# Fused attention, experts and MLP on one core: the attention's work put in another order on three engines

## The chip, the cores and the metric

One core of one Trainium2 chip runs the whole program. The metric is the device time of one execution in microseconds (us); lower is better. TensorE multiplies and transposes, ScalarE (ACT) and VectorE (DVE) read its results from the eight PSUM banks, GpSimd (POOL) works on SBUF, and SyncE (SP) issues all DMAs. Each engine works through its own list of instructions in the order in which they are written.

## The reference

```
def sm_attn(qq, kk, vv):
    s = scale * np.matmul(qq, kk.transpose(0, 1, 3, 2))
    s = s - np.max(s, axis=-1, keepdims=True)
    a = np.exp(s)
    a = a / (np.sum(a, axis=-1, keepdims=True) + 1e-09)
    return np.matmul(a, vv)
p_packed = sm_attn(p, k, v)              # 32 packed queries per head
out = sm_attn(q, p_packed, p_packed)     # q, k, v: (4, 8, 576, 64)
...
x = out as (2304, 512); logits = x @ w_gate; P = exp(logits), 8 rounds of row and column scaling
out += P[:, e:e+1] * (relu(x @ w1[e]) @ w2[e])    # 8 experts, hidden 1024
h = x @ w_in; r = relu(h); out = (s * r * r + b) @ w_out   # hidden 2048
```

## The kernel before

Attention goes batch by batch, b = 0 to 3, and two batches are in flight at any time. All that TensorE has to turn round (transpose) is cut into *units*, and a unit fills one PSUM bank: `("p", b, 0)` the packed queries; `("k", b, 0..5)` and `("q", b, 0..5)` four heads by one chunk of tokens each (the third chunk is a short tail); `("e", b, 0..2)` the exponentials of the first softmax; `("pp", b, 0)` the packed values; `("a", b, 0..2)` the weights of the second softmax, which are the attention's result for the experts. The list `UNITS` holds their order. Unit n goes to bank `TR[n % 3]`, and TensorE may write it only when unit n-3 has been copied out (`wait_evacuated(pe, [unit - 3])` in `transposes`). So three units are in flight, and one late copy holds up every turn that follows.

Between the turns stand the products of each batch, in this order of need: `scores1(b, Q)` (packed queries by keys, Q = 0, 1); VectorE's `max1`; ScalarE's `exp1`; `turn_e`; `packed(b)` (80 small matmuls, weights by values); VectorE's `inverse1` and `normalise1`; `turn_packed`; ScalarE's `packed_values`; `scores2(b, c)` for three chunks c; VectorE's `off_max2`; ScalarE's `exp2`; VectorE's `inverse2`; GpSimd's `normalise2`; `turn_a(b, c)`; and `a_chunk(b, c)` on ScalarE (high part) and then on VectorE (low part). `packed_gates`, `gates_of_packed`, `lo_of_packed` and `first_products` prepare gate logits and the first expert group. After the attention comes `hidden(0, 0, 0, 0)` and a long part that is the same in both kernels: 32 expert groups and 8 MLP groups.

The order is written out by hand, once for each engine: the calls in the TensorE block, those in the ScalarE block, those in the VectorE block, and `order_of_units()`, with one pattern for b = 1 and 2. `BY_ACT` fixes who copies: ScalarE copies every unit but `("k", b, 3)`. SyncE loads `q[b + 1]`, the packed queries and `k[b + 2]` when the last unit of `q[b]` has been turned, and `v[b + 1]` after `packed(b)`.

Of the kernel before, what the change touches and what calls it, by code (L numbers as in the profile page):

```python
# [12 lines left out]
P = 128  # L13
# [5 lines left out]
def attention_moe_mlp(nc, q, k, v, p, w_gate, w1, w2, w_in, w_out, s_, b_, out):  # L19
    B, H, S, D = q.shape  # L20
    NPACK = p.shape[2]
# [34 lines left out]
    with ExitStack() as ctx:  # L56
# [127 lines left out]
        ppT_ready = sem("ppT_ready")  # L184
# [103 lines left out]
        def order_of_units():  # L288

            def parts(what, b, some):  # L290
                return [(what, b, n) for n in some] if 0 <= b < B else []
            order = parts("k", 0, range(3)) + parts("p", 0, [0]) + parts("k", 0, range(3, 6)) + parts("q", 0, range(6))
            order += parts("e", 0, range(3)) + parts("pp", 0, [0]) + parts("p", 1, [0])
            order += parts("k", 1, range(6)) + parts("q", 1, range(6))
            for b in range(1, B - 1):
                order += parts("e", b, range(3)) + parts("p", b + 1, [0]) + parts("k", b + 1, range(3))
                order += parts("pp", b, [0]) + parts("k", b + 1, range(3, 6)) + parts("a", b - 1, [0])
                order += parts("q", b + 1, range(4)) + parts("a", b - 1, [1])
                order += parts("q", b + 1, [4, 5]) + parts("a", b - 1, [2])
            order += parts("e", B - 1, range(3)) + parts("a", B - 2, [0]) + parts("pp", B - 1, [0])  # L300
            order += parts("a", B - 2, [1, 2])
            order += parts("a", B - 1, range(NC))
            return order

        UNITS = order_of_units()

        BY_ACT = [("p", 0), ("k", 0), ("k", 1), ("k", 2), ("k", 4), ("k", 5), ("q", 0), ("q", 1), ("q", 2), ("q", 3),
                  ("q", 4), ("q", 5), ("e", 0), ("e", 1), ("e", 2), ("pp", 0)]
# [115 lines left out]
        def _(sp):  # L424
# [55 lines left out]

            for b in range(B - 1):
# [141 lines left out]
        def _(act):  # L623
# [24 lines left out]
            def evacuate(what, b, part, dst, view):  # L648
                assert (what, part) in BY_ACT
                unit = UNITS.index((what, b, part))  # L650
                copy(dst, view(full(unit))).then_inc(evacuated(unit), 1)
# [12 lines left out]
            def a_chunk(b, c):  # L664

                if b < 0:
                    return
                copy(out_cols(a_hi, b, c), turned_a(full(UNITS.index(("a", b, c))), c)).then_inc(a_hi_ready, 1)

            def packed_values(b):  # L670

                i, unit = b % 2, UNITS.index(("pp", b, 0))
                src = full(unit)[:, 0:QUADS * P]
                copy(ppT[i][:], src).then_inc(ppT_ready, 1)
                copy(pp_parts[0:HALF, :, b * NPACK:(b + 1) * NPACK],
                     src[0:HALF, :].rearrange("d (h n) -> d h n", n=NPACK)).then_inc(evacuated(unit), 1)

            def p_part(b):
                if b < B:
                    evacuate("p", b, 0, pT[b % 2][:], lambda bank_: bank_[:, 0:QUADS * P])  # L680

            def k_part(b, n):
                if b == B:
                    return
# [8 lines left out]
            def q_part(b, n):  # L693
                if b < B:
                    evacuate("q", b, n, *queries_of(b, n))

            k_part(0, 0)
            k_part(0, 1)  # L700
            k_part(0, 2)
            p_part(0)
            k_part(0, 4)
            exp1(0, 0)
            k_part(0, 5)
            q_part(0, 0)
            exp1(0, 1)
            for n in range(1, UNITS_IN):
                q_part(0, n)
            for n in range(3):  # L710
                evacuate("e", 0, n, *turned_e(0, n))
            packed_values(0)
            p_part(1)
            exp2(0, 0)
            k_part(1, 0)
            k_part(1, 1)
            k_part(1, 2)
            exp2(0, 1)
            exp1(1, 0)
            k_part(1, 4)  # L720
            k_part(1, 5)
            exp2(0, 2)
            q_part(1, 0)
            exp1(1, 1)
            for n in range(1, UNITS_IN):
                q_part(1, n)
            for b in range(1, B):
                for n in range(3):
                    evacuate("e", b, n, *turned_e(b, n))
                if b == B - 1:  # L730
                    a_chunk(b - 1, 0)
                    packed_values(b)
                    a_chunk(b - 1, 1)
                    a_chunk(b - 1, 2)
                    break
                p_part(b + 1)
                for n in range(3):
                    k_part(b + 1, n)
                packed_values(b)
                exp1(b + 1, 0)  # L740
                k_part(b + 1, 4)
                k_part(b + 1, 5)
                a_chunk(b - 1, 0)
                exp2(b, 0)
                q_part(b + 1, 0)
                exp1(b + 1, 1)
                q_part(b + 1, 1)
                q_part(b + 1, 2)
                exp2(b, 1)
                q_part(b + 1, 3)  # L750
                a_chunk(b - 1, 1)
                exp2(b, 2)
                q_part(b + 1, 4)
                q_part(b + 1, 5)
                a_chunk(b - 1, 2)
# [16 lines left out]

            first_hi_part(0, 0)
            exp2(B - 1, 0)
            first_hi_part(1, 0)
            exp2(B - 1, 1)
            relu(0, 0, 0, 0)
            exp2(B - 1, 2)
            relu(0, 0, 0, 1)
            first_hi_part(0, 1)  # L780
            first_hi_part(1, 1)
            relu(0, 0, 1, 0)
# [69 lines left out]
        def _(dve):  # L852
# [14 lines left out]
            def evacuate(what, b, part, dst, view):  # L867
                assert (what, part) not in BY_ACT
# [31 lines left out]
            def inverse2(b, c):  # L900
                if b < 0:
                    return
# [6 lines left out]
            def a_chunk(b, c):  # L909

                if b < 0:
                    return
# [6 lines left out]
            def k_part(b, n):  # L919
                if b < B:  # L920
                    evacuate("k", b, n, *keys_of(b, n))

            def lo_of_packed(b):
                unit = UNITS.index(("pp", b, 0))
                wait_evacuated(dve, [unit])
# [12 lines left out]

            max1(0, 0)
            k_part(0, 3)  # L940
            max1(0, 1)
            inverse1(0)
            normalise1(0)
            off_max2(0, 0)
            inverse2(0, 0)
            off_max2(0, 1)
            max1(1, 0)
            k_part(1, 3)
            lo_of_packed(0)
            inverse2(0, 1)  # L950
            off_max2(0, 2)
            dve.wait_ge(wg_ready, 2)
            gates_of_packed(0)
            max1(1, 1)
            inverse2(0, 2)
            inverse1(1)
            for b in range(1, B):
                normalise1(b)
                if b == B - 1:
                    for c in range(NC):  # L960
                        a_chunk(b - 1, c)
                    break
                max1(b + 1, 0)
                k_part(b + 1, 3)
                off_max2(b, 0)
                a_chunk(b - 1, 0)
                max1(b + 1, 1)
                inverse2(b, 0)
                off_max2(b, 1)
                gates_of_packed(b)  # L970
                a_chunk(b - 1, 1)
                off_max2(b, 2)
                inverse2(b, 1)
                inverse2(b, 2)
                a_chunk(b - 1, 2)
                inverse1(b + 1)
                lo_of_packed(b)
# [99 lines left out]

            last = B - 1
            off_max2(last, 0)
            first_lo_part(0, 0)  # L1080
            off_max2(last, 1)
            first_lo_part(1, 0)
            off_max2(last, 2)
            inverse2(last, 0)
            lo_of_packed(last)
            gates_of_packed(last)
            inverse2(last, 1)
            lo_of_hidden(0, 0, 0, 0)
            inverse2(last, 2)
            lo_of_hidden(0, 0, 0, 1)  # L1090
            first_lo_part(0, 1)
            first_lo_part(1, 1)
            lo_of_hidden(0, 0, 1, 0)
            lo_of_hidden(0, 0, 1, 1)
# [81 lines left out]
        def _(pe):  # L1176
# [24 lines left out]
            def turn_p(b):  # L1201
                if b < B:
                    pe.wait_ge(p_in[b % 2], (b // 2 + 1) * 32)
# [24 lines left out]
            def scores1(b, Q):  # L1228
                if b == B:
                    return  # L1230
# [77 lines left out]
            def turn_a(b, c):  # L1308
                if b < 0:
                    return  # L1310
# [327 lines left out]
```

## Time and profile before

| | |
|---|---|
| Time, median of 3 (lowest to highest) | 1775.69 us (1770.3 to 1777.31) |
| The profiled execution: its time, its span | 1775.83 us, 1774.0 us |
| TensorE busy (matmul), share of the span | 1752.3 us, 99% |
| VectorE, ScalarE, GpSimd busy | 913.3, 713.2, 609.4 us |
| Granted TensorE clock, mean | 0.991 |

The time is the span plus 1.8 us around it. Busy time of an engine is the time in which the profile has an instruction on it. For TensorE the ends are modelled, so a stretch that is full of matmuls need not run at its peak, but a gap is a gap. The granted clock is 1.00 at 2.4 GHz and 0.50 at 1.2 GHz. The attention takes the first 100 us of the span.

### The profile page before, as it was taken

The numbers are of one execution on the slowest core, as the hardware profiler recorded it, in microseconds if no ns is written. First come the engines' busy times: TensorE is split into PE (matmuls) and PEld (weight loads), VectorE is DVE, ScalarE is ACT, GpSimd is POOL, SyncE is SP. The second block draws the span as 40 slices with busy tenths as digits, with TensorE's granted clock in tenths as the row PEclk, the third lists the DMA queues.
The fourth block names the chain that finished last, engine by engine and source line by source line (L and its number), as shares of the span: only waits on it lengthen the run. The fifth ranks groups of instructions, "written<-read, shape, count | busy, mean of one in ns | idle before, by whom it ended". The sixth has DMA issues, their size and how long they took to land.

```text
span 1774.0 us, 27319 instructions
## 1 busy us (share of the span) xinstructions
PE 1752.3 (99%) x10257; PEld 1525.5 (86%) x10257; DVE 913.3 (51%) x1361; ACT 713.2 (40%) x1574; POOL 609.4 (34%) x380
## 2 busy tenths in 40 slices
PE   8899999999999999999999999999999999999999
PEld 6688888898889888888988898889888888888887
DVE  3555654544544554455445544544556555555555
ACT  4543446345444434443454345444432322222222
POOL 1153444443444444345344443444431011111100
PEclk8899999999999999999999999999999999999999
DMA  7531112111111121111112111111100000000002
GB/s 218 152 72 37 36 36 59 37 47 37 35 36 35 46 48 35 47 35 35 35 35 59 36 45 37 35 35 36 47 24 24 13 24 25 25 24 24 0 0 106
DMA packets 71776, 78.81 MB, mean 44 GB/s; under 512 B 7984, under 2 KB 59184, under 8 KB 71728
## 3 DMA queue, kind: packets, MB, share of 16 engines
q1 hardware_dynamic: 71728, 78.15, 16.6%
q8 instruction: 33, 0.54, 0.1%
q14 instruction: 15, 0.12, 0.0%
HBM read 73.42 MB, written 4.72 MB: 44 GB/s over the span
## 4 chain that ended last, share of the span: by engine, by line
PE 96%; DVE 2%; ACT 1%; issue 0%; DVEq 0%
PE PS L1178 94%; PE PS L1198 1%; DVE acc L1035 1%; PE PS L1473 0%; DVE gate L1012 0%; ACT acc L625 0%; ACT g_raw L625 0%; DVE stat L896 0%; DVE gate L998 0%; DVE stat L905 0%; DVE a_parts L915 0%; DVE stat L906 0%; DVE stat L875 0%; ACT a_parts L625 0%; DVE acc L897 0%
## 5 line engine op out<-in xcount | busy, mean ns | idle before, releaser
L1178 PE MATMUL PS<-w_hi,h_hi 128*128 128x512 f32 x1440 | 563.5, 391 | 1.3 <-DVE acc L1035 1.3
L1178 PE MATMUL PS<-w_hi,h_lo 128*128 128x512 f32 x1440 | 561.0, 390 | 0.0
L1178 PE MATMUL PS<-w_lo,h_hi 128*128 128x512 f32 x1440 | 560.7, 389 | 0.0
L1040 DVE SCALAR_TENSOR_TENSOR acc<-PS,gate,acc 128x512 f32<-128x512 f32 x504 | 378.0, 750 | 266.9 <-PE PS L1178 266.9
L764 ACT ACTIVATE h_hi<-PS 128x576 fp32r<-128x576 f32 x256 | 167.1, 653 | 676.6 <-PE PS L1178 675.9
L1178 PE MATMUL PS<-a_parts,g_parts 128*128 128x288 f32 x3072 | 438.0, 295 | 0.6 <-DVE g_parts L983 0.6
L1178 PEld LDWEIGHTS PS<-a_parts,g_parts 128*128 128x128 f32 x3072 | 419.4, 188 | 6.0 <-DVE g_parts L983 0.7
L625 ACT ACTIVATE g_raw<-PS 32x256 f32<-32x256 f32 x992 | 373.3, 376 | 14.3 <-PE PS L1178 0.4
L1021 DVE SCALAR_TENSOR_TENSOR h_lo<-PS,h_hi 128x576 fp32r<-128x576 f32 x256 | 193.9, 757 | 324.9 <-ACT h_hi L764 324.9
L1178 PEld LDWEIGHTS PS<-w_hi,h_hi 128*128 128x128 f32 x1440 | 270.3, 188 | 57.5 <-DVE acc L1035 3.9
L1178 PEld LDWEIGHTS PS<-w_hi,h_lo 128*128 128x128 f32 x1440 | 270.3, 188 | 57.5
L1178 PEld LDWEIGHTS PS<-w_lo,h_hi 128*128 128x128 f32 x1440 | 270.4, 188 | 52.8
L542 POOL CAST w_hi<-stage 128x1024 fp32r<-128x1024 f32 (+1 forms) x78 | 77.0, 987 | 381.5 <-PE PS L1178 374.8
L565 POOL CAST g_parts<-g_raw 128x1024 fp32r<-128x1024 f32 x62 | 64.6, 1042 | 390.1 <-ACT g_raw L625 390.1
L544 POOL TENSOR_TENSOR w_lo<-stage,w_hi 128x1024 fp32r<-128x1024 f32 (+1 forms) x78 | 169.9, 2179 | 6.2
L1035 DVE TENSOR_TENSOR acc<-PS,acc 128x512 f32<-128x512 f32 x180 | 124.2, 690 | 54.0 <-PE PS L1178 53.2
L567 POOL TENSOR_TENSOR g_parts<-g_raw,g_parts 128x1024 fp32r<-128x1024 f32 x62 | 148.8, 2400 | 5.0
L836 ACT ACTIVATE mlp_f<-PS 128x512 f32<-128x512 f32 (+1 forms) x80 | 44.5, 556 | 219.9 <-PE PS L1178 219.9
L1178 PE MATMUL PS<-a_parts,w_hi 128*128 128x512 f32 (+1 forms) x320 | 117.9, 368 | 0.0
L1178 PE MATMUL PS<-a_parts,w_lo 128*128 128x512 f32 (+1 forms) x320 | 117.7, 368 | 0.0
L1178 PE MATMUL PS<-g_parts,w_hi 128*128 128x512 f32 (+1 forms) x320 | 117.7, 368 | 0.0
L557 POOL CAST w_hi<-stage 128x1024 fp32r<-128x1024 f32 x40 | 41.7, 1042 | 201.5 <-PE PS L1178 197.1
(127 smaller groups left out, 1086.3 us busy)
## 6 DMA issues: line engine op xcount, KB each, us to landing
stage<-moe_w_dram SPq DMA_DIRECT2D x96, 512.0 KB, 5.0
k_raw<-k_dram SPq DMA_DIRECT2D x8, 512.0 KB, 6.1
q_raw<-q_dram SPq DMA_DIRECT2D x8, 512.0 KB, 5.7
v_raw<-v_dram SPq DMA_DIRECT2D x8, 512.0 KB, 6.1
stage<-moe_w_in_dram SPq DMA_DIRECT2D x16, 256.0 KB, 2.9
stage<-moe_w_out_dram SPq DMA_DIRECT2D x8, 512.0 KB, 3.4
out_dram<-acc SPq DMA_DIRECT2D x16, 256.0 KB, 2.2
p_twice<-p_dram SPq DMA_DIRECT2D x8, 64.0 KB, 4.8
```

Source lines behind the costliest of these rows:

```text
L542: nc.gpsimd.tensor_copy(hi, src).then_inc(w1_ready, 1)
L544: nc.gpsimd.tensor_tensor(lo, src, hi.bitcast(F32), ALU.subtract).then_inc(w1_ready, 1)
L557: nc.gpsimd.tensor_copy(w2_hi[par][:], stage2[:]).then_inc(w2_ready, 1)
L565: nc.gpsimd.tensor_copy(g_hi[par][:, Q], g_raw[Q][:]).then_inc(g_hi_ready, 1)
L567: nc.gpsimd.tensor_tensor(g_lo[par][:, Q], g_raw[Q][:], g_hi[par][:, Q].bitcast(F32), ALU.subtract).then_inc(g_lo_ready, 1)
L625: return nc.scalar.activation(dst, src, ACT.Copy)
L764: nc.scalar.activation(dst.rearrange("p (i n) -> p i n", i=2), src, ACT.Relu).then_inc(h_hi_ready, 1)
L836: nc.scalar.activation(mlp_f[:, slot, f, 0:n], bank(HB + 2 * slot + f, n), ACT.Relu).then_inc(relu_ready, 1)
L1021: nc.vector.scalar_tensor_tensor(out=h_lo[:, f, cols].rearrange("p (i n) -> p i n", i=2), in0=bank(HB + 2 * f, 2 * BANK).rearrange("p (i n ...
L1035: return nc.vector.tensor_tensor(dst, y, dst, ALU.add)
L1040: return nc.vector.scalar_tensor_tensor(out=dst, in0=y, scalar=share, in1=dst, op0=ALU.mult, op1=ALU.add)
L1178: return nc.tensor.matmul(dst, lhsT, rhs, start=start, stop=stop)
```

## The change

Nothing that is computed changes, nor how often. The hand-made patterns go. In their place stand four lists, each for all four batches: `TURNED_UNITS` (the order in which banks are filled), the calls of TensorE, those of ScalarE and those of VectorE. Copies are shared out anew: VectorE keeps units k13, k23 and k33 and also copies k00, k04, q02, q00, e01, q05, k15, e11 and k22 (letter, batch, part); ScalarE takes k03. The high part of the packed values is copied from SBUF in a call of its own, `hi_of_packed`, later in ScalarE's list. Waits are finer: `scores1(b, Q)` waits for its own three key units, `scores2(b, c)` for the packed values and for the two query units of its chunk. SyncE waits apart for the turned packed queries and keys. `first_products(0, 0)` and `(1, 0)` move ahead of the last batch's `scores2`, `packed_gates(3)` behind the first `hidden`.

```diff
+        TURNED_UNITS = """
+            p00 k00 k02 k01 k05 k03 k04 q02 q03 e00 q00 e01 e02 q01 q04 q05 p10 k12 k11 pp00 k10 k13
+            k14 k15 q15 q12 q13 q10 k20 q14 k25 e10 q11 e11 e12 k23 k21 p20 k22 k24 q25 pp10 a00 q23
+            q24 q22 a01 q21 e20 e21 e22 q20 p30 a02 k32 k31 k30 k34 pp20 k33 a10 k35 q35 q30 a11 q31
+            e30 e31 q32 e32 q33 q34 a12 a20 pp30 a21 a22 a30 a31 a32
+        """.split()
+        UNITS = [(name[:-2], int(name[-2]), int(name[-1])) for name in TURNED_UNITS]
...
             for b in range(B - 1):
-                sp.wait_ge(tr_full, UNITS.index(("q", b, UNITS_IN - 1)) + 1)
+                wait_turned("q", b)
                 load(q_raw[0], q[b + 1], q_in)
                 if b + 2 < B:
+                    wait_turned("p", b)
                     load_queries(b + 2)
+                    wait_turned("k", b)
                     load(k_raw[b % 2], k[b + 2], k_in[b % 2])
...
+            def hi_of_packed(b):
+                wait_evacuated(act, [UNITS.index(("pp", b, 0))])
                 copy(pp_parts[0:HALF, :, b * NPACK:(b + 1) * NPACK],
-                     src[0:HALF, :].rearrange("d (h n) -> d h n", n=NPACK)).then_inc(evacuated(unit), 1)
+                     ppT[b % 2][0:HALF, :].rearrange("d (h n) -> d h n", n=NPACK)).then_inc(pp_hi_ready, 1)
...
-                wait_evacuated(pe, [UNITS.index(("p", b, 0))] + [UNITS.index(("k", b, j)) for j in range(NC * Q + NC)])
+                wait_evacuated(pe, [UNITS.index(("p", b, 0))] + [UNITS.index(("k", b, j))
+                                                                 for j in range(NC * Q, NC * Q + NC)])
...
-                if c == 0:
-                    pe.wait_ge(ppT_ready, b + 1)
-                    wait_evacuated(pe, [UNITS.index(("q", b, j)) for j in range(UNITS_IN)])
+                wait_evacuated(pe, [UNITS.index(("pp", b, 0))] + [UNITS.index(("q", b, QUADS * c + Q))
+                                                                  for Q in range(QUADS)])
```

**TensorE, around the end of batch 0.** In the rows below `acc` and `second` are the SBUF space of even and odd batches. `ident,acc 128x128` are turns of exponentials or of second weights, `128x64` is `turn_a(0, 2)`. Before, the last part of the stretch from `packed(1)` to `packed(2)`:

```order
L1198 MATMUL PS<-ident,q_raw 128x128 x8
L1198 MATMUL PS<-ident,acc 128x128 x4
L1178 MATMUL PS<-ppT,second 32x32 x16
L1198 MATMUL PS<-ident,q_tail 128x32 x8
L1198 MATMUL PS<-ident,acc 128x64 x2
L1198 MATMUL PS<-ident,acc 128x128 x8
L1198 MATMUL PS<-ident,acc 64x128 x2
L1198 MATMUL PS<-ident,p_twice 128x128 x2
L1198 MATMUL PS<-ident,k_raw 128x128 x4
```

Now, also up to `packed(2)`:

```order
L1241 MATMUL PS<-ident,q_raw 128x128 x4
L1221 MATMUL PS<-wg_raw,ppT 32x8 x8
L1221 MATMUL PS<-acc,pT 32x288 x8
L1241 MATMUL PS<-ident,acc 128x128 x4
L1221 MATMUL PS<-ppT,second 128x128 x16
L1241 MATMUL PS<-ident,acc 128x128 x4
L1241 MATMUL PS<-ident,acc 64x128 x2
L1241 MATMUL PS<-ident,q_raw 128x128 x4
L1241 MATMUL PS<-ident,p_twice 128x128 x2
L1241 MATMUL PS<-ident,acc 128x64 x2
```

A wide `scores2(1, 1)` (`ppT,second`, 16 matmuls) now stands between the first and the second turn of exponentials, and the second `scores1(2, 1)` (`acc,pT`) just ahead of them; the narrow `scores2(1, 2)` has gone behind `packed(2)`.

**VectorE, the same stretch.** L915 and L926 are the low part of a turned second weight (`a_chunk`), which frees a bank. L905 to L907 and L918 to L920 are `inverse2`. Before:

```order
L915 TENSOR_TENSOR a_parts<-PS,a_parts 128x2x256
L896 TENSOR_REDUCE stat_1<-PS 64x8
L897 TENSOR_TENSOR second<-PS,stat_1 64x256
L905 TENSOR_REDUCE stat_1<-second 128x16
L906 TENSOR_SCALAR stat_1<-stat_1 128x16
L907 RECIPROCAL stat_1<-stat_1 128x16
L905 TENSOR_REDUCE stat_1<-second 64x8
L906 TENSOR_SCALAR stat_1<-stat_1 64x8
L907 RECIPROCAL stat_1<-stat_1 64x8
L915 TENSOR_TENSOR a_parts<-PS,a_parts 128x2x64
```

Now:

```order
L926 TENSOR_TENSOR a_parts<-PS,a_parts 128x2x256
L955 CAST gw_high<-PS 128x2x8
L956 CAST gw_both<-PS 128x2x8
L957 TENSOR_TENSOR gw_both<-PS,gw_high 128x2x8
L918 TENSOR_REDUCE stat_0<-acc 64x8
L919 TENSOR_SCALAR stat_0<-stat_0 64x8
L920 RECIPROCAL stat_0<-stat_0 64x8
L911 TENSOR_REDUCE stat_1<-PS 128x16
L912 TENSOR_TENSOR second<-PS,stat_1 128x512
L926 TENSOR_TENSOR a_parts<-PS,a_parts 128x2x64
```

The `inverse2` calls of batch 1 have left the space ahead of `a_chunk(0, 2)`; one `inverse2` of batch 0 and one `off_max2` of batch 1 stand there now.

**TensorE, the end of the attention.** `stage,pp_parts` is `first_products`, `a_parts,g_parts` is `hidden`, `wg_raw,ppT` is `packed_gates`. Before:

```order
L1198 MATMUL PS<-ident,acc 128x64 x2
L1178 MATMUL PS<-ppT,second 128x128 x16
L1178 MATMUL PS<-stage,pp_parts 32x256 x8
L1178 MATMUL PS<-ppT,second 128x128 x16
L1178 MATMUL PS<-stage,pp_parts 32x256 x8
L1178 MATMUL PS<-ppT,second 32x32 x16
L1178 MATMUL PS<-wg_raw,ppT 32x8 x8
L1178 MATMUL PS<-a_parts,g_parts 128x288 x24
```

Now:

```order
L1221 MATMUL PS<-stage,pp_parts 32x256 x16
L1241 MATMUL PS<-ident,acc 128x128 x4
L1241 MATMUL PS<-ident,acc 128x64 x2
L1221 MATMUL PS<-ppT,second 128x128 x32
L1221 MATMUL PS<-ppT,second 32x32 x16
L1221 MATMUL PS<-a_parts,g_parts 128x288 x12
L1221 MATMUL PS<-wg_raw,ppT 32x8 x8
L1221 MATMUL PS<-a_parts,g_parts 128x288 x12
```

The first products come before the last turns and scores, and nothing stands any more between the last scores and the first `hidden`.

## Rows read from the trace of the kernel before

**Rows 1.** The page, busy time of each engine

```profile
PE 1752.3 (99%) x10257; PEld 1525.5 (86%) x10257; DVE 913.3 (51%) x1361; ACT 713.2 (40%) x1574; POOL 609.4 (34%) x380
```

**Rows 2.** Busy time by stretch, the attention in five parts of 20 us

```profile
core 0: us, PE busy (x) PEld busy (x) DVE busy (x) ACT busy (x) POOL busy (x), PEclk, DMA share, GB/s
0.00:20.00 20.00, 15.72 (x160) 12.70 (x164) 2.92 (x8) 9.25 (x22) 2.49 (x8) 0.93 0.95 280
20.00:40.00 20.00, 16.79 (x240) 13.39 (x233) 10.68 (x28) 8.71 (x23) 2.71 (x3) 0.81 0.50 156
40.00:60.00 20.00, 18.01 (x295) 13.94 (x293) 9.46 (x22) 11.00 (x27) 1.05 (x1) 0.91 0.63 190
60.00:80.00 20.00, 18.54 (x251) 14.36 (x252) 9.99 (x25) 9.64 (x26) 2.73 (x3) 0.74 0.74 195
80.00:100.00 20.00, 16.16 (x294) 12.36 (x291) 11.29 (x28) 8.28 (x20) 5.07 (x4) 0.83 0.01 2
```

**Rows 3.** TensorE in order of time: start us, us, idle before and releaser

```profile
23.22 3.79 PE L1178 MATMUL PS<-ppT,acc 64*128 64x128 f32 x32
...
34.88 0.72 PE L1178 MATMUL PS<-second,pT 64*32 64x288 f32 x16 [0.57 <-ACT second L625]
...
42.53 1.08 PE L1178 MATMUL PS<-v_raw,second 128*32 128x64 f32 x32
...
43.91 0.93 PE L1178 MATMUL PS<-v_raw,second 128*32 128x64 f32 x32
...
45.02 0.66 PE L1198 MATMUL PS<-ident,k_raw 128*128 128x128 f32 x4
...
46.70 0.72 PE L1178 MATMUL PS<-acc,pT 64*32 64x288 f32 x16 [0.29 <-ACT acc L625]
47.36 1.09 PE L1198 MATMUL PS<-ident,k_raw 128*128 128x128 f32 x8
...
48.74 2.06 PE L1178 MATMUL PS<-ppT,second 64*128 64x128 f32 x32
...
59.01 0.31 PE L1198 MATMUL PS<-ident,acc 64*128 64x64 f32 x2 [0.81 <-DVE a_parts L915]
60.39 1.06 PE L1198 MATMUL PS<-ident,acc 128*128 128x128 f32 x8 [1.08 <-ACT acc L625]
62.41 0.61 PE L1198 MATMUL PS<-ident,acc 128*64 128x128 f32 x2 [0.95 <-DVE a_parts L915]
...
63.24 1.06 PE L1198 MATMUL PS<-ident,k_raw 128*128 128x128 f32 x4
64.23 1.08 PE L1178 MATMUL PS<-v_raw,acc 128*32 128x64 f32 x32
...
100.44 3.45 PE L1178 MATMUL PS<-a_parts,g_parts 128*128 128x288 f32 x24 [0.62 <-DVE g_parts L983]
```

**Rows 4.** Busy time by stretch, the four in which the clock stood at 0.5

```profile
17.30:27.50 10.20, 8.73 (x122) 6.93 (x121) 1.05 (x3) 1.94 (x6) 0.00 (x0) 0.50 1.09 334
...
41.50:44.90 3.40, 3.40 (x85) 2.64 (x84) 0.00 (x0) 1.11 (x3) 0.00 (x0) 0.55 1.05 322
...
61.90:71.90 10.00, 9.37 (x121) 6.68 (x122) 2.83 (x10) 3.46 (x10) 0.63 (x1) 0.50 0.55 163
...
85.60:92.40 6.80, 5.67 (x92) 4.19 (x92) 2.33 (x9) 1.86 (x5) 1.97 (x4) 0.50 0.01 2
```

**Rows 5.** VectorE in order of time: first maximum, copy of a unit, second maximum

```profile
47.53 0.76 DVE L875 TENSOR_REDUCE stat<-PS 128x1 f32<-128x576 f32 x1 [1.69 <-PE PS L1178]
...
48.39 0.68 DVE L870 COPY acc<-PS 128x512 f32<-128x512 f32 x1
...
50.84 0.69 DVE L896 TENSOR_REDUCE stat<-PS 128x16 f32<-128x512 f32 x1 [1.76 <-PE PS L1178]
```

**Rows 6.** ScalarE in order of time: copy of a unit, first exponential

```profile
42.64 0.60 ACT L625 ACTIVATE acc<-PS 128x512 f32<-128x512 f32 x1 [0.62 <-PE PS L1198]
...
48.51 0.74 ACT L656 ACTIVATE acc<-PS,stat 128x576 f32<-128x576 f32 x1 [1.34 <-DVE stat L876]
```

More of the change, by code:

```diff
@@ L693, in q_part, with e_part @@
             def q_part(b, n):
[L694 to L755, printed above, removed]
+                evacuate("q", b, n, *queries_of(b, n))
+            def e_part(b, n):
+                evacuate("e", b, n, *turned_e(b, n))
             def relu_chunk(g, u, half, f):
@@ L771, in scale @@
                                          ).then_inc(acc_scaled, 1)
+            p_part(0)
+            k_part(0, 2)
+            k_part(0, 1)
+            k_part(0, 5)
+            k_part(0, 3)
+            exp1(0, 0)
+            q_part(0, 3)
+            exp1(0, 1)
+            e_part(0, 0)
+            e_part(0, 2)
+            q_part(0, 1)
+            q_part(0, 4)
+            p_part(1)
+            k_part(1, 2)
+            k_part(1, 1)
+            packed_values(0)
+            k_part(1, 0)
@@ new lines, in _ @@
+            hi_of_packed(0)
+            k_part(1, 4)
+            q_part(1, 2)
+            exp1(1, 0)
+            q_part(1, 5)
+            q_part(1, 3)
+            exp2(0, 0)
+            q_part(1, 0)
+            k_part(2, 0)
+            exp1(1, 1)
+            q_part(1, 4)
+            k_part(2, 5)
+            e_part(1, 0)
+            q_part(1, 1)
+            exp2(0, 1)
+            e_part(1, 2)
+            k_part(2, 1)
+            p_part(2)
+            k_part(2, 4)
+            q_part(2, 5)
@@ new lines, in _ @@
+            packed_values(1)
+            a_chunk(0, 0)
+            q_part(2, 4)
+            exp2(0, 2)
+            q_part(2, 3)
+            exp1(2, 0)
+            q_part(2, 2)
+            hi_of_packed(1)
+            a_chunk(0, 1)
+            e_part(2, 0)
+            exp1(2, 1)
+            q_part(2, 1)
+            e_part(2, 1)
+            e_part(2, 2)
+            q_part(2, 0)
+            a_chunk(0, 2)
+            exp2(1, 0)
+            exp2(1, 1)
+            p_part(3)
+            k_part(3, 2)
@@ new lines, in _ @@
+            k_part(3, 1)
+            k_part(3, 0)
+            k_part(3, 4)
+            packed_values(2)
+            a_chunk(1, 0)
+            exp2(1, 2)
+            k_part(3, 5)
+            exp1(3, 0)
+            q_part(3, 5)
+            q_part(3, 0)
+            a_chunk(1, 1)
+            hi_of_packed(2)
+            q_part(3, 1)
+            exp1(3, 1)
+            exp2(2, 0)
+            e_part(3, 0)
+            e_part(3, 1)
+            e_part(3, 2)
+            exp2(2, 1)
+            q_part(3, 3)
@@ L937, in gates_of_packed @@
                                         ALU.subtract).then_inc(gw_ready, 1)
[L939 to L977, printed above, removed]
             def first_lo_part(Q, late):
@@ L1092, in _ @@
-            first_lo_part(1, 1)
-            lo_of_hidden(0, 0, 1, 0)
-            lo_of_hidden(0, 0, 1, 1)
+            k_part(0, 0)
+            max1(0, 0)
+            k_part(0, 4)
+            q_part(0, 2)
+            max1(0, 1)
+            q_part(0, 0)
+            e_part(0, 1)
+            q_part(0, 5)
+            inverse1(0)
+            normalise1(0)
+            k_part(1, 3)
+            k_part(1, 5)
+            max1(1, 0)
+            off_max2(0, 0)
+            dve.wait_ge(wg_ready, 2)
@@ new lines, in _ @@
+            gates_of_packed(0)
+            max1(1, 1)
+            inverse2(0, 0)
+            off_max2(0, 1)
+            inverse1(1)
+            e_part(1, 1)
+            k_part(2, 3)
+            inverse2(0, 1)
+            normalise1(1)
+            k_part(2, 2)
+            lo_of_packed(0)
+            off_max2(0, 2)
+            a_chunk(0, 0)
+            max1(2, 0)
+            off_max2(1, 0)
+            max1(2, 1)
+            a_chunk(0, 1)
+            gates_of_packed(1)
+            inverse2(0, 2)
@@ new lines, in _ @@
+            off_max2(1, 1)
+            a_chunk(0, 2)
+            inverse1(2)
+            inverse2(1, 0)
+            normalise1(2)
+            inverse2(1, 1)
+            off_max2(1, 2)
+            max1(3, 0)
+            k_part(3, 3)
+            a_chunk(1, 0)
+            inverse2(1, 2)
+            lo_of_packed(1)
+            off_max2(2, 0)
+            max1(3, 1)
+            a_chunk(1, 1)
+            gates_of_packed(2)
+            off_max2(2, 1)
+            inverse2(2, 0)
+            off_max2(2, 2)
@@ new lines, in _ @@
+            inverse1(3)
+            inverse2(2, 1)
+            normalise1(3)
+            inverse2(2, 2)
+            a_chunk(1, 2)
+            a_chunk(2, 0)
+            lo_of_packed(2)
+            first_lo_part(0, 0)
+            a_chunk(2, 1)
+            a_chunk(2, 2)
+            first_lo_part(1, 0)
+            off_max2(3, 0)
+            off_max2(3, 1)
+            off_max2(3, 2)
+            lo_of_packed(3)
+            gates_of_packed(3)
+            inverse2(3, 0)
+            lo_of_hidden(0, 0, 0, 0)
@@ L1095, in _ @@
+            inverse2(3, 1)
+            lo_of_hidden(0, 0, 0, 1)
+            inverse2(3, 2)
+            first_lo_part(0, 1)
+            lo_of_hidden(0, 0, 1, 0)
+            first_lo_part(1, 1)
+            lo_of_hidden(0, 0, 1, 1)
+            last = B - 1
             for t in range(UT):
@@ L1342, in first_products @@
                 pe.wait_ge(pp_split, 2 * late + 2)
+                pe.wait_ge(e1_ready, B * QUADS)
+                if late:
+                    wait_evacuated(pe, range(LAST - 3, LAST))
+                    pe.wait_ge(s2_taken, (B - 1) * NC + 2)
+                    pe.wait_ge(gw_ready, 2 * B)
                 n, dst, _, _ = first_of(Q, late)
@@ L1504, in weights @@
                         for Q in range(QUADS)]
-            last_batch, batches = B - 1, (B - 1) * NC
-            scores2(last_batch, 0)
+            turn_p(0)
+            turn_k(0, 0)
+            turn_k(0, 2)
+            turn_k(0, 1)
+            turn_k(0, 5)
+            turn_k(0, 3)
+            scores1(0, 0)
+            turn_k(0, 4)
+            turn_q(0, 2)
+            scores1(0, 1)
+            turn_q(0, 3)
+            turn_e(0, 0)
+            turn_q(0, 0)
+            turn_e(0, 1)
@@ new lines, in _ @@
+            turn_e(0, 2)
+            turn_q(0, 1)
+            turn_q(0, 4)
+            turn_q(0, 5)
+            packed(0)
+            turn_p(1)
+            turn_k(1, 2)
+            turn_k(1, 1)
+            turn_packed(0)
+            turn_k(1, 0)
+            turn_k(1, 3)
+            packed_gates(0)
+            turn_k(1, 4)
+            scores1(1, 0)
+            turn_k(1, 5)
+            turn_q(1, 5)
+            turn_q(1, 2)
+            scores2(0, 0)
+            turn_q(1, 3)
+            scores1(1, 1)
@@ new lines, in _ @@
+            turn_q(1, 0)
+            turn_k(2, 0)
+            turn_q(1, 4)
+            scores2(0, 1)
+            turn_k(2, 5)
+            turn_e(1, 0)
+            turn_q(1, 1)
+            turn_e(1, 1)
+            turn_e(1, 2)
+            scores2(0, 2)
+            turn_k(2, 3)
+            turn_k(2, 1)
+            packed(1)
+            turn_p(2)
+            turn_k(2, 2)
+            turn_k(2, 4)
+            turn_q(2, 5)
+            turn_packed(1)
+            scores1(2, 0)
+            turn_a(0, 0)
@@ new lines, in _ @@
+            turn_q(2, 3)
+            turn_q(2, 4)
+            scores2(1, 0)
+            turn_q(2, 2)
+            turn_a(0, 1)
+            turn_q(2, 1)
+            packed_gates(1)
+            scores1(2, 1)
+            turn_e(2, 0)
+            scores2(1, 1)
+            turn_e(2, 1)
+            turn_e(2, 2)
+            turn_q(2, 0)
+            turn_p(3)
+            turn_a(0, 2)
+            packed(2)
+            turn_k(3, 2)
+            turn_k(3, 1)
+            turn_k(3, 0)
+            scores2(1, 2)
@@ new lines, in _ @@
+            turn_k(3, 4)
+            turn_packed(2)
+            scores1(3, 0)
+            turn_k(3, 3)
+            turn_a(1, 0)
+            turn_k(3, 5)
+            scores2(2, 0)
+            turn_q(3, 5)
+            turn_q(3, 0)
+            turn_a(1, 1)
+            scores1(3, 1)
+            turn_q(3, 1)
+            packed_gates(2)
+            scores2(2, 1)
+            turn_e(3, 0)
+            turn_e(3, 1)
+            turn_q(3, 2)
+            turn_e(3, 2)
+            scores2(2, 2)
@@ L1508, in _ @@
+            turn_q(3, 3)
+            packed(3)
+            turn_q(3, 4)
+            turn_a(1, 2)
+            turn_a(2, 0)
+            turn_packed(3)
             first_products(0, 0)
-            scores2(last_batch, 1)
             first_products(1, 0)
-            scores2(last_batch, 2)
-            pe.wait_ge(s2_taken, batches + 2)
-            packed_gates(last_batch)
+            turn_a(2, 1)
+            turn_a(2, 2)
+            scores2(3, 0)
+            scores2(3, 1)
+            scores2(3, 2)
@@ L1514, in _ @@
             pe.wait_ge(first_split, 2)
             hidden(0, 0, 0, 0, weights(0, 0, 0, 0), (a_hi, a_lo))
[L1516 removed]
+            packed_gates(3)
+            pe.wait_ge(s2_taken, (B - 1) * NC + 3)
             hidden(0, 0, 0, 1, weights(0, 0, 0, 1), (a_hi, a_lo))
             first_products(0, 1)
[L1519 removed]
             first_products(1, 1)
```

172 lines of the change are left out of this document (40 added, 132 removed).

## The prediction

> **What bounds the kernel now.** I read the page's busy times first: TensorE has 1752.3 of 1774.0 us, the others about half [rows 1]. After the attention TensorE works nearly without a gap on instructions that the change does not touch. So the change can only move the point at which the first `hidden` starts, 100.44 us [rows 3], and what moves there moves the end by as much.
>
> The view by stretch says what there is to win. TensorE is busy for 15.72, 16.79, 18.01, 18.54 and 16.16 us of five times 20 [rows 2], so it is idle for 4.28 + 3.21 + 1.99 + 1.46 + 3.84 = 14.8 us, and 0.62 more just before `hidden` [rows 3]: 15.4 us. VectorE and ScalarE are busy for about half of every stretch [rows 2]. No engine besides TensorE is short of time; TensorE waits because the right copy or maximum is not the next one in another engine's list.
>
> The second loss is the clock. In four stretches it stands at 0.5, the 1.2 GHz level: 17.3 to 27.5, 41.5 to 44.9, 61.9 to 71.9 and 85.6 to 92.4 us, with 27.2 us of busy time [rows 4]. Ahead of the last two falls TensorE had gaps of about 1 us between short turns; those ahead of the third can be read: 0.81, 1.08 and 0.95 us [rows 3].
>
> **What the steps of TensorE take.** At the full level, from start to start: `scores1` 0.66 us (46.70 to 47.36), a unit of four 128x128 turns 0.51 (eight turns last 1.09, with 0.07 of overhang), a wide `scores2` 1.99 [rows 3]. At the half level: `scores2` 3.79 for 2.06, four turns 0.99 (63.24 to 64.23) for 0.51; half of `packed` 1.38 (42.53 to 43.91), against 1.11 for the other half, nearly all at the full level [rows 3]. So `packed` costs 2.76 or 2.2. The small steps are estimates from these rows by their columns: a tail unit 0.36, two turns 0.25 to 0.3, a narrow `scores2` 0.63, `packed_gates` 0.23. One batch has 8 large and 4 tail units of keys and queries (5.5), p 0.3, two `scores1` 1.3, e 1.3, `packed` 2.2, pp 0.3, `scores2` 4.6, gates 0.2, a 1.3: 17.0 us at the full level. From `packed(1)` at 42.53 to `packed(2)` at 64.23, one batch's worth, it is now 21.7 [rows 3].
>
> **The change, part by part.** The instructions are the same but for some more semaphore waits. The copies that go from ScalarE to VectorE take 0.68 instead of 0.60 us [rows 5, 6]; nine of them add 6 us to VectorE's 44, which has the room [rows 2]. What counts is the order. I went through the four new lists by hand with the durations above, an end-to-reader delay of 0.70 us from the start of a four-turn unit, 0.98 for `max1` with its scaling, 0.84 for `exp1`, 1.46 for `off_max2`; these last are the row durations [rows 5, 6] and a small step each.
>
> *Start to `packed(0)`.* Packed queries are now turned first, which may wait some 0.3 us for their load. `scores1(0, 1)` still waits for `exp1(0, 0)`: about 1.0 us idle; `turn_e(0, 1)` about 0.55 for ScalarE. With 1.06 us before the first instruction and 0.2 in small ones some 3.1 us of idle stay. `packed(0)` comes at 16.6 us, some 1.8 earlier.
>
> *Batch 0's second softmax.* Before, `scores1(1, 1)` waited 0.57 us for ScalarE [rows 3], and most turns behind it followed ScalarE. Now `scores2(0, 0)` stands between the two `scores1(1, .)`, so `max1(1, 0)` and `exp1(1, 0)` run beneath it (1.99 us over 0.98 + 0.84). I find no wait over 0.1 us up to `packed(1)`.
>
> *`packed(1)` to `packed(2)`, the pattern of the rest.* Before, 2.84 us are lost at 59 to 62.4 [rows 3]: `turn_a(0, 2)`, `turn_e` and the last e unit stand together, each unit's bank waits for the copy of the third unit before, and `a_chunk` on VectorE stands behind `inverse2(1, 0)` and `(1, 1)`. Now `scores2(1, 1)` covers `exp1(2, 1)` and the low part of `a_chunk(0, 1)`, and `inverse2(1, .)` comes after `a_chunk(0, 2)`. The tightest places are `pp10`, which waits for VectorE's k22 behind `normalise1(1)` (0.4 us), and p30 (0.1). The same holds one batch on, where the last stretch has 3.84 us of idle [rows 2].
>
> *The end.* The two early `first_products` cover the turns of a21 and a22, and `hidden` stands right behind `scores2`: its 0.62 us go. `packed_gates(3)` waits for `off_max2(3, 1)`, which has the 3.45 us of `hidden` [rows 3] to finish in. `inverse2(3, 2)` is late, behind ScalarE's last `first_hi_part`, but its turn is far back in `outputs`. The load of the next group's weights and the way to its first product are as long as before.
>
> *Idle, in sum:* 15.4 - 3.1 = 12.3 us removed. The new waits in the first part of `scores2` and the finer ones of `scores1` cost nothing, since TensorE is then late and the semaphore has passed.
>
> *The clock.* Of the 27.2 us at the half level about 10.4 are `packed` (three at 2.76 and three quarters of one), which would save a fifth, 2.1. The other 16.8 would save at most half, 8.4, and at least the 1.7 of `scores2(0, 0)` and 0.5 for each unit of turns, some 3.5 in all; I take 6.4, together 8.5. The first stretch (2.7 of these) follows turns and gaps before 17.3 us that mostly stay, so I keep its cost. The other three followed gaps that go: 5.8 us, between 0 and 5.8.
>
> **The sum.** -12.3 - 5.8 = -18.1. I give back 2 us for hand-overs that a walk does not see: the same sums for the kernel before (5.7 for the start, 69.7 of work, 14.3 later idle, 8.5 for the clock) come to 98.2 for 100.44. And 2 us for one more half-level stretch like the second or fourth, 3.4 to 6.8 us, at half its length or less. -14 on the profiled execution's 1775.8, which stands 0.1 from the median of the runs: **1762 us**.
>
> On stalls of this sort the Trainium skill ("TensorE: Matmul & The Clock Gate", the section on psum-queue depth-cycling) says that matmul groups that cycle through PSUM banks with small idles in between make the clock swing between its levels. The new order still cycles through three banks. By that rule the 5.8 us would not come, and the sum would be about 1768; in this trace the falls that can be read came after gaps near 1 us, and between 44.9 and 61.9 us the same cycling ran at the full level.
>
> **The rivals.**
> *A: the waits move instead of going* (0.13). Each list has places at which an engine stands before something not yet there: VectorE reaches `max1(2, 1)` with its scores still a us away, with `a_chunk(0, 1)`, which frees a bank, behind it. If each batch loses 1.5 us so, and the gaps bring one or two half-level stretches back, 6 and 4 us return: 1766 to 1771, taken as 1769.
> *B: data comes late* (0.05). The tail of `q[2]` is wanted some 5.5 us after its load can be issued, and the profile has no row of a load beside this timing. Against it: in the kernel before, all later loads came well ahead. 1 to 2 us in each of three batches: 1767 on its own, 1770 with lost clock.
> *C: the clock stays at the half level* (0.05), slower. The new order mixes turns and short products everywhere. If the half level, once there at 17.3 us, held to the end of the attention, the 60 us of work left after it (8.8 of it `packed`) would take 11 + 51 x 1.9 = 108 us, where it now takes 83: 1775.8 + 25 less 0.6 for the rest, 1800. A us of work done at the half level costs about 0.9 more, so a us spent there costs 0.47. The 12.3 us of idle are eaten up by 26 us there beyond the 30.4 of now: it decides from about 57 us on.
> *D: the gain is lost further on* (0.02): a GpSimd split or DMA that becomes the limit of group 1. 1775.
>
> **How the numbers follow.** The forecast has 0.75, and its own range is 1755 (no allowance, and the first half-level stretch gone too: -18.1 - 2.7) to 1767. For 8 in 10 I go to 1769.5 above and stay at 1755 below. A measurement of this kernel can tell about 0.5%, 8.9 us, from no change, so faster means below 1766.8: the forecast's 0.75 and 0.03 of A. The rest of A, B and D: 0.17 the same. C: 0.05 slower.
>
> **What would show it.** The first `hidden` at 84 to 89 us instead of 100.44; `packed(0)` near 16.6, `packed(2)` near 54; TensorE idle for 3 to 5 us up to there; stretches with the clock at 0.5 of 10 to 17 us in all instead of 30.4. The same distance as before from `hidden` to the end. Wrong would be: waits of 1 us or more at turns for VectorE, a first `hidden` after 92, or a granted clock at 0.5 through a whole `scores2` in batches 1 to 3.

## The result, and the profile after

The changed kernel takes 1751.82 us (median of 4 runs, 1751.18 to 1752.34); the one before, on the same chip, 1772.99 (1770.14 to 1777.31). The ratio is 0.9878, 95% interval 0.9853 to 0.9904: 21.2 us or 1.2% faster. The forecast was 1762, with a range from 1755: the direction was right, the size too small by a third, and the range missed. The profiled execution went from a span of 1774.0 us to 1749.4, by 24.6.

The page's busy times:

```profile
PE 1739.2 (99%) x10257; PEld 1516.6 (87%) x10257; DVE 916.5 (52%) x1371; ACT 710.0 (41%) x1564; POOL 609.1 (35%) x380
```

TensorE has the same 10257 matmuls as in [rows 1] and is busy for 13.1 us less. That is the first surprise: gaps that close don't shorten busy time. The view by stretch, as in [rows 2]:

```profile
0.00:20.00 20.00, 17.09 (x208) 13.77 (x208) 6.40 (x15) 8.75 (x21) 2.48 (x8) 1.00 0.95 278
20.00:40.00 20.00, 19.51 (x333) 15.04 (x331) 11.99 (x32) 11.42 (x28) 2.10 (x2) 1.00 0.88 269
40.00:60.00 20.00, 19.88 (x350) 16.03 (x348) 15.56 (x40) 14.01 (x35) 3.55 (x4) 1.00 0.79 232
60.00:80.00 20.00, 19.80 (x379) 16.53 (x380) 17.73 (x45) 11.27 (x24) 6.77 (x6) 1.00 0.21 44
...
0.00:75.54 75.54, 71.81 (x1211) 57.52 (x1211) 47.46 (x118) 43.49 (x104) 14.24 (x19) 1.00 0.75 218
75.54:1749.40 1673.86, 1667.40 (x9052) 1459.09 (x9047) 869.08 (x1254) 666.50 (x1461) 594.81 (x361) 1.00 0.14 37
```

The clock is 1.00 everywhere: none of the four stretches of [rows 4] is left. The same view of the kernel before up to its first `hidden` reads:

```profile
0.00:100.44 100.44, 85.22 (x1227) 66.76 (x1227) 44.78 (x110) 47.06 (x115) 14.04 (x19) 0.85 0.56 164
```

The first `hidden` starts at 75.54 us instead of 100.44, 24.9 us earlier, and from there to the end both kernels need the same time within 0.3 us. The 24.9 split into idle, 100.44 - 85.22 = 15.2 before and 75.54 - 71.81 = 3.7 now, so 11.5 us; and busy time, 85.2 against 71.8, so 13.4 us. Of these 0.2 are a `packed_gates` that now comes later; the other 13.2 are the same work done at a higher clock. TensorE in order of time:

```profile
6.95 0.43 PE L1241 MATMUL PS<-ident,k_tail 32*128 32x32 f32 x4 [0.37 <-DMA k_tail<-k_dram]
...
11.62 0.72 PE L1221 MATMUL PS<-acc,pT 64*32 64x288 f32 x16 [0.81 <-ACT acc L647]
...
14.34 0.97 PE L1241 MATMUL PS<-ident,acc 128*128 128x128 f32 x6 [0.54 <-ACT acc L647]
...
16.45 0.65 PE L1221 MATMUL PS<-v_raw,acc 128*32 128x64 f32 x32
...
18.11 0.44 PE L1241 MATMUL PS<-ident,p_twice 128*128 128x128 f32 x2
...
20.66 0.66 PE L1241 MATMUL PS<-ident,k_raw 128*128 128x128 f32 x4 [0.49 <-DMA k_raw<-k_dram]
...
34.26 0.65 PE L1221 MATMUL PS<-v_raw,second 128*32 128x64 f32 x32
...
48.94 0.65 PE L1221 MATMUL PS<-v_raw,acc 128*32 128x64 f32 x32
...
65.23 0.65 PE L1221 MATMUL PS<-v_raw,second 128*32 128x64 f32 x32
...
67.53 0.31 PE L1241 MATMUL PS<-ident,second 64*128 64x64 f32 x2 [0.20 <-issue]
...
75.54 1.85 PE L1221 MATMUL PS<-a_parts,g_parts 128*128 128x288 f32 x12
```

With the 1.06 us at the start these are all the gaps of 0.2 us or more, and after 21 us there is one. The three of [rows 3] at 59 to 62 us have no successor. `packed(0)` takes 1.66 us (16.45 to 18.11); the prediction had put it at 2.2 from a row in which the clock was just changing.

### The profile page after: what moved, and what is told of

The parts are those of the page before. It is cut to its first block, busy times and chain, and to the rows that moved or that the text cites. A ratio compares the mean times of both kernels' runs of the same rounds, so it can differ in the third digit from the quotient of the medians.

```text
span 1749.4 us, 27331 instructions
## 1 busy us (share of the span) xinstructions
PE 1739.2 (99%) x10257; PEld 1516.6 (87%) x10257; DVE 916.5 (52%) x1371; ACT 710.0 (41%) x1564; POOL 609.1 (35%) x380
## 3 DMA queue, kind: packets, MB, share of 16 engines
q1 hardware_dynamic: 71728, 78.15, 16.6%
## 4 chain that ended last, share of the span: by engine, by line
PE 97%; DVE 1%; SPq 1%; DMA 0%; ACT 0%; issue 0%; DVEq 0%
PE PS L1221 95%; PE PS L1241 1%; DVE acc L1016 1%; DMA k_raw<-k_dram 0%; PE PS L1455 0%; DVE gate L993 0%; SPq L413 0%; ACT g_raw L617 0%; DVE gate L979 0%; SPq L437 0%; SPq L430 0%; SPq L418 0%; PE PS L1425 0%; DVE col_sum L983 0%; DVE row_inverse L976 0%
## 5 line engine op out<-in xcount | busy, mean ns | idle before, releaser
L1190 DVE SCALAR_TENSOR_TENSOR mlp_f<-mlp_f,s_and_b 128x512 f32<-128x512 f32 (+1 forms) x80 | 58.6, 733 | 100.4 <-ACT mlp_f L852 100.3
```

Of the source, the lines that this page charges most:

```text
L1190: nc.vector.scalar_tensor_tensor(out=r, in0=r, scalar=s_and_b[:, 0:1], in1=r, op0=ALU.mult, op1=ALU.mult).then_inc(f_ready, 1)
```

## The experiments

All times are medians. The kernel before was timed again beside each group, at 1770.8 to 1775.6 us; e9, e10 and e0 are one group, on another chip.

**e1: the finer waits alone.**

```diff
-  ... for j in range(NC * Q + NC)])
+  ... for j in range(NC * Q, NC * Q + NC)])
-  if c == 0:
-      pe.wait_ge(ppT_ready, b + 1)
-      wait_evacuated(pe, [UNITS.index(("q", b, j)) for j in range(UNITS_IN)])
+  pe.wait_ge(ppT_ready, b + 1)
+  wait_evacuated(pe, [UNITS.index(("q", b, QUADS * c + Q)) for Q in range(QUADS)])
```

> The kernel before with the finer waits alone (scores1 waits for its own three key units, each scores2 for its own two query units); all orders as before. If the order is what pays: within 2 us of the kernel before, since where TensorE waited before, it waited at turns. If the finer waits pay: 5 us or more faster.

1775.83 us, ratio 1.0003 (0.999 to 1.0015). The finer waits give nothing by themselves. Its profiled execution happened to be a short one, and by stretch, up to the time of before's first `hidden` and up to its own, it reads:

```profile
0.00:100.44 100.44, 84.96 (x1287) 67.18 (x1288) 50.33 (x127) 49.80 (x120) 16.95 (x22) 0.93 0.56 164
...
0.00:94.45 94.45, 78.97 (x1226) 62.28 (x1226) 44.67 (x110) 47.00 (x115) 14.02 (x19) 0.93 0.60 174
```

Here the first `hidden` came at 94.45, 6.0 us before that of the kernel before, with some 14 us at the half level instead of 30. Its idle time up to there is 94.45 - 78.97 = 15.5 us, against 15.2 in the kernel before. The same instructions in the same order with the same waits, and the clock alone moves them by 6 us.

**e3: the copies given back to ScalarE** (k00, k04, q02, q00, e01, q05, k15, e11, k22), each behind the unit before it; TensorE's order as in the changed kernel.

```diff
             # ScalarE's list
             p_part(0)
+            k_part(0, 0)
             k_part(0, 2)
...
             # VectorE's list
-            k_part(0, 0)
             max1(0, 0)
-            k_part(0, 4)
-            q_part(0, 2)
             max1(0, 1)
```

> The changed kernel with the nine copies that VectorE took over given back to ScalarE, each right behind the unit before it; TensorE's order unchanged. If the order alone pays: within 2 us of the changed kernel, 22 to 25 us under the kernel before. If the new share of copies pays too: gaps of 0.3 to 0.6 us behind those units, 3 to 6 us in all, and perhaps a half-level stretch again, so 5 to 12 us of the gain gone.

1753.03 us, 1.2 over the changed kernel; two of its four runs are at 1751.8. The profiled one has this view of waits and, by stretch, one fall of the clock:

```profile
PE PS L1221 <- ACT acc L647: 1.5, 1, 1.5
```

```profile
9.90:13.30 3.40, 3.23 (x25) 1.79 (x24) 0.91 (x2) 1.33 (x3) 0.00 (x0) 0.52 1.09 347
```

One wait, for the first exponential, has grown from 0.81 to 1.50 us, and this stretch at half clock lies ahead of it. What stands ahead of the stretch is a wait for a load, which the profiled execution of the changed kernel does not have:

```profile
9.33 0.76 PE L1241 MATMUL PS<-ident,k_raw 128*128 128x128 f32 x4 [0.80 <-DMA k_raw<-k_dram]
```

The expected gaps of 0.3 to 0.6 us behind the moved units do not show. So the order gives nearly all. The 1.2 us of the median are no proof for the new share of copies: two runs are level with the changed kernel, and in the profiled one the loss begins with data that came late.

**e8: the end of the attention as before.**

```diff
-            first_products(0, 0)
-            first_products(1, 0)
             turn_a(2, 1)
             turn_a(2, 2)
             scores2(3, 0)
+            first_products(0, 0)
             scores2(3, 1)
+            first_products(1, 0)
             scores2(3, 2)
+            packed_gates(3)
             pe.wait_ge(first_split, 2)
             hidden(0, 0, 0, 0, weights(0, 0, 0, 0), (a_hi, a_lo))
-            packed_gates(3)
```

> The changed kernel with the end of the attention as before: first_products between the last scores2, packed_gates ahead of the first hidden. If the end's order gave its share of 0.6 to 0.9 us: the first hidden waits 0.6 us again and a turn or scores2 a little, 0.6 to 2 us over the changed kernel in all. If the order of the middle gave everything: within 0.3 us of it.

1753.50 us, 1.7 over the changed kernel (lowest run 1.3 over its lowest). Its first `hidden`:

```profile
76.84 3.33 PE L1221 MATMUL PS<-a_parts,g_parts 128*128 128x288 f32 x23 [0.52 <-DVE g_parts L964]
```

That is 1.3 us later than 75.54: the wait is back with 0.52 us, `a_chunk` brings another of 0.51 at 68.4, and 0.24 are `packed_gates`. This execution was 0.7 us ahead before its end part began, since `packed(3)` starts at 64.53 instead of 65.23. From there to the first `hidden` it takes 12.31 us against 10.31, so the end's order is worth 1.7 us by the medians and 2.0 by the profiles, where the prediction had named 0.62.

**e2 and e9: the gaps filled, nothing else.** The question was what the 13 us of clock come from. In the kernel before, TensorE multiplies the constant tile `ones` where it would wait; nothing reads the result. The diff is e9's; e2 has fewer of them, in bank 7.

```diff
+            def fill(count):
+                for _ in range(count):
+                    mm(bank(5, P), ones[:], ones[:])
...
             for b in range(1, B):
                 for n in range(3):
+                    if b > 1 and n != 1:
+                        fill(4)
                     turn_e(b, n)
...
                 turn_q(b + 1, 5)
+                fill(3)
                 turn_a(b - 1, 2)
```

> The kernel before, in whose gaps TensorE multiplies a constant tile that nothing reads (31 products of 128 columns, some 0.23 us each at 2.4 GHz); orders, copies and waits as before. It removes no wait. If the half-level stretches come from the gaps: the clock stays at 1.00 in all or nearly all of the attention, and 9 to 13 us go although not one gap is won back. If they come from the mix of turns and short products, or from chance: 30 us at the half level as before, and a time equal or up to 3 us longer.

e2 has 41 such products (the expectation miscounted). It took 1768.81 us, ratio 0.9965 (0.9952 to 0.9978), 6.8 us less than the kernel before, with two short half-level stretches left:

```profile
21.70:25.20 3.50, 3.40 (x27) 2.92 (x28) 0.00 (x0) 0.92 (x3) 0.00 (x0) 0.53 1.09 323
35.20:38.60 3.40, 3.38 (x27) 2.24 (x28) 1.15 (x3) 0.73 (x3) 0.00 (x1) 0.55 0.00 0
```

The first stands behind gaps of 0.81 and 0.93 us that it had not filled, the second behind a wait of 2.03 us that one of its fillings made itself, since it waited for VectorE. e9 mends this and fills the remaining gaps, with 51 products in all (again more than the expectation counted).

> The kernel before with products that nothing reads in all of its gaps (46 of 128 columns), none of which waits for anything; e2_fill had still two falls, one behind a wait of 2 us that its filling had made itself. If the clock's part of the gain is 13 us and gaps are its cause: clock at 1.00 throughout, 1761 to 1765 us, that is 10 us or more under the kernel before with its waits all still there. If the clock's part is the 8.5 us of the prediction: 1766 to 1769 us. If the falls have another cause: they stay, over 1772 us.

1767.46 us, ratio 0.9978 (0.9967 to 0.9989) to the kernel before beside it (1770.97). The stretch up to its first `hidden`:

```profile
0.00:91.46 91.46, 85.55 (x1329) 70.04 (x1329) 44.78 (x110) 46.84 (x115) 14.04 (x19) 1.00 0.61 180
```

The clock is 1.00, and the first `hidden` comes 9.0 us earlier than in the kernel before though no wait has been taken away. It was not the 1761 to 1765 that I expected, since the filling costs more than the gaps. Within a group a product takes 0.23 us, which makes 11.7 for 51, but a group also costs time at its ends: the busy time of 85.55 is 13.5 above the 72.05 that the same work takes in the changed kernel (71.81 and the 0.24 of `packed_gates`). With the 5.9 us of idle that remain this makes 19.4 where there were 15.2. So the clock gave 11.3 us if the filling is put at 11.7, and 13.2 if it is put at 13.5.

**e4, e5, e6, e10: gaps put into the changed kernel.** ScalarE gets additional copies ahead of those on which TensorE waits.

```diff
+            def idle(at, n):      # n * 128 columns, to a place that is free until the experts
+                copy(w1_hi[:, at * P:(at + n) * P].rearrange("p (o d) -> p o d", d=P),
+                     ones[:].unsqueeze(1).to_broadcast([P, n, P]))
...
+            idle(0, 16)           # e4; 32 in e5
             e_part(3, 0)
```

> The changed kernel with one additional ScalarE copy of 2048 columns (about 2 us) ahead of its copy of e30, which opens one gap of some 1.9 us on TensorE at 64 us. If a gap costs only itself: 1.5 to 2.5 us over the changed kernel and the clock at 1.00. If a gap of that size also brings the half level: 4 to 7 us over it, with a stretch at 0.5 behind the gap.

e4: 1752.07 us, 0.25 over the changed kernel. ScalarE had been idle for 1 us ahead of that copy and had finished it early, so 2 us of work left a gap of 0.63 only. The clock stayed at 1.00. My estimate of the gap was wrong; the row gave the slack.

> The changed kernel with about 4.1 us of additional ScalarE copies ahead of its copy of e30; the 2 us of the earlier run left a gap of 0.63 us, so now one of some 2.7 us. If the half level follows from gaps whose sum is like that of before: 2.7 us and 1.5 to 3 us of clock, so 4 to 6 us over the changed kernel, a stretch at 0.5 behind the gap. If a gap costs only itself: 2.5 to 3 us over it, clock at 1.00.

e5: 1755.29 us, 3.5 over; one of the four runs kept a mean clock of 1.000 and took 1753.2. TensorE in order of time:

```profile
66.54 0.60 PE L1250 MATMUL PS<-ident,second 128*64 128x128 f32 x2 [2.42 <-ACT second L617]
67.07 1.07 PE L1230 MATMUL PS<-ppT,acc 64*32 64x32 f32 x32
68.07 1.11 PE L1250 MATMUL PS<-ident,q_raw 128*128 128x128 f32 x4
```

Right behind a gap of 2.42 us the narrow `scores2` takes 1.07 instead of 0.69 us, the four turns 1.11 instead of 0.66: the half level, from 66.3 to 69.6 us. 2.4 us are the gap, 1.1 the clock.

> The changed kernel with the same additional ScalarE work in three pieces, ahead of its copies of e21, e22 and q20: three gaps of near 1 us within 5 us, as the kernel before had them at 59 to 62 us. If the clock follows from such gaps: a fall right behind them, 10 us or less at 0.5, 4.5 to 7 us over the changed kernel. If gaps cost only themselves: 3 us over it.

e6: 1755.97 us, 4.2 over. Only two gaps came:

```profile
48.79 0.41 PE L1252 MATMUL PS<-ident,p_twice 128*128 128x128 f32 x2 [0.41 <-ACT acc L617]
50.39 0.31 PE L1252 MATMUL PS<-ident,acc 64*128 64x64 f32 x2 [1.19 <-ACT acc L617]
```

```profile
51.20:58.20 7.00, 6.87 (x114) 5.56 (x114) 3.93 (x13) 4.48 (x12) 2.10 (x2) 0.52 1.05 298
```

1.6 us of gaps, then 7 us at the half level: the fall costs more than the gaps. One of the four runs kept a mean clock of 1.000 and took 1753.7. e10 is e6 with seven products of `ones` in the two gaps.

> e6_three_gaps, whose two gaps (0.41 and 1.19 us) cost 4.2 us over the changed kernel with 7 us at the half level behind them; here TensorE multiplies a constant tile in both. If the fall came from the gaps: clock at 1.00, 1.5 to 2.2 us over the changed kernel. If the additional ScalarE work costs it in another way: 4 us over it as before.

e10: 1755.54 us, 4.0 over the changed kernel beside it (1751.55). The clock of the profiled execution is 1.00 with the same additional ScalarE work, so the fall came from the gaps. The time is not the expected 1.5 to 2.2: the additional ScalarE work opens a gap of 0.89 us at k31 besides, and two of 0.7 us, put down to issue, stand at 65 and 71 us. What e6 paid in clock, e10 pays in gaps and in the filling, some 2 us of each up to the first `hidden`; for the price of a fall this run says nothing, and where the two issue gaps come from stays open.

**e7: k01 turned ahead of the tail k02.**

```diff
-            p00 k00 k02 k01 k05 k03 k04 ...
+            p00 k00 k01 k02 k05 k03 k04 ...
```

> The changed kernel with k01 turned ahead of the tail k02, for which TensorE waited 0.37 us. If the start is the limit of what follows it: the first scores1 0.4 to 0.6 us earlier and the whole kernel as much faster. If the waits for the first exponentials take it up again, or the next load does: no difference.

1752.18 us, no difference. The wait at the tail goes, but the first `scores1` starts at 8.87 us instead of 8.85, and `scores1(0, 1)` waits 0.79, where it was 0.81. The eight turns of k00 and k01 now take 1.45 us from start to start, where the kernel before has 1.03 for eight such turns at 9.23 us; why they are slow is open.

**e0: the changed kernel once more.**

> The changed kernel unchanged, on the chip of the two others, as their measure: 1751 to 1753 us, clock at 1.00.

1751.55 us (1751.34 to 1752.58), ratio 0.9889 (0.9873 to 0.9905) to the kernel before beside it. No version that I ran beats it.

**The runs of the kernel before as an experiment.** Its 39 further runs, on two chips, span 1766.0 to 1775.6 us, at a mean clock from 0.997 to 0.989. The averages lie near a line; five of the nine clock values that occur are:

| Mean clock | 0.997 | 0.996 | 0.994 | 0.991 | 0.989 |
|---|---|---|---|---|---|
| Runs | 3 | 5 | 9 | 11 | 1 |
| Span, us | 1766.2 | 1767.4 | 1769.1 | 1774.1 | 1775.6 |

A straight line through all 39 gives 0.38 us for each us at the half level and a span of 1761.6 at clock 1.00; the three groups of runs by themselves give 0.36 to 0.38 and 1761.4 to 1762.0. None of the runs reached 1.00, so the 1761.6 is read off beyond them. So of the profiled 24.6 us the clock is 1774.0 - 1761.6 = 12.4 and the waits are 1761.6 - 1749.4 = 12.2. The changed kernel's 9 runs all have a mean clock of 1.0 and lie within 1.4 us.

## Why the prediction was right, and where it was wrong

*Waits: right.* The step "15.4 - 3.1 = 12.3 us removed" measured 11.5 by the gaps and 12.2 by the line. The four gaps that it left standing are there: 1.06 before the first instruction, 0.37 for a load (said 0.3), 0.81 for `exp1(0, 0)` (said 1.0), 0.54 for the first exponentials (said 0.55); `packed(0)` came at 16.45 (said 16.6). `packed(2)`, said to come near 54, came at 48.94. It missed one of 0.49 for k13, whose load comes late, and foresaw one at pp10 that did not come. Rival A (the waits move) and B (late data, beyond that 0.49) did not happen, and C, the clock, went the other way.

*The clock: wrong in three terms.* The step "The sum" took 5.8 us for it and gave 4 back, where 12 to 13 us came.
- "I take 6.4, together 8.5": all four stretches cost 12.4 (the line), 13.2 (busy time) or 11.3 to 13.2 (e9) and not 8.5. The price of `packed` at the full level was the clearest error: 2.2 was read from a half that ran from 43.91 to 45.02, "nearly all at the full level", while [rows 4] has the half level until 44.9. It is 1.66, so each half-level `packed` of 2.76 cost 1.1 us and not 0.56, in all 4.1 and not 2.1. By the line the other 16.8 us then cost 8.3, nearly the whole of the 8.4 that the prediction had as their most, and not 6.4.
- "The first stretch (2.7 of these) follows turns and gaps before 17.3 us that mostly stay, so I keep its cost": it went as well. In the changed kernel gaps of 0.81 and 0.54 us are there, yet all 9 runs have a mean clock of 1.0. But the gaps had not mostly stayed: TensorE's idle time between 5 and 17.3 us went from 2.6 to 1.85 us, and the longest gap of the kernel before in it is gone:

```profile
15.34 0.89 PE L1198 MATMUL PS<-ident,q_tail 32*128 32x32 f32 x8 [1.09 <-ACT acc L625]
```

- "-14" with 2 us for one more half-level stretch and 2 for unseen hand-overs: neither came. The sum for the kernel before fell 2.2 us short for another reason than hand-overs. Its four `packed` at 2.2 made the work 2.2 us too long, and its clock of 8.5 was 3.9 too short; with both put right it gives 99.9 for 100.44.

With 12.4 in the place of 5.8 and without the 4 the sum is -24.7; 24.6 was measured between the two profiled executions. By the medians it was 21.2, since the profiled execution of the kernel before was one of its slower ones. The low end of the range was made of the same 8.5, so it could not hold it.

*The cause of the falls* was argued from their place behind gaps. e9 (gaps filled, clock up), e5 and e6 (gaps opened, clock down) and e10 (the same gaps filled, clock up) show it. The Trainium skill ("TensorE: Matmul & The Clock Gate", psum-queue depth-cycling) ties the swinging of the clock to small idles between groups of matmuls that cycle through banks. The prediction read it as a price of the cycling: that is not borne out, since the same three banks cycle for 75 us at the full level. The idles are, by e9 and e6. What decides whether a given gap brings a fall stays open; one and the same kernel falls in some runs and not in others.

*The change part by part.* Order: nearly all. Share of copies: at most about 1 us, and not shown (e3). End: 1.7 to 2.0 us (e8), said 0.62. Finer waits alone: nothing (e1). Two things were not tested: whether the new order needs the finer waits, and which engine's new order gives how much.

## What to carry to other kernels

Where TensorE is the bound and waits in short gaps, look at its clock in the same stretches: gaps of about 1 us can cost as much again through the half level that follows them (here 12 us and 12 us). Take the full-level duration of a step only from a row that lies wholly in a stretch at 1.00, and cost a us at the half level at about 0.4 us of time, as measured here. When several engines share one ring of buffers, a product of 2 us between a link of the softmax and the turn that needs it is worth trying; this order has such products, and no run tested one of them apart.

## What I had not expected of the hardware

- The spread of a kernel's runs can be its clock: 39 runs of one program from 1766.0 to 1775.6 us of span, in a line with the mean granted clock.
- The kernel can be made faster by TensorE work that nobody needs: 41 extra products took 0.35% off the time of the kernel before (e2), 51 of them 0.22% (e9).
- 0.41 and 1.19 us of gap were followed by 7 us at 1.2 GHz (e6), 2.42 us by 3.3 us (e5), and 0.81 and 0.54 us (changed kernel) or 0.89 us (e10) by none.
